# Short remainders of experts taken out of the tile loop into one mixed tile of plain 32-bit matmuls

## The reference

```python
logits = x @ w_gate + modality_bias[modality_id]
e_idx = np.argmax(logits, axis=1)
gate_w = probs[np.arange(N), e_idx]          # softmax of the logits at the chosen expert
for e in range(8):
    mask = e_idx == e
    h = np.maximum(x[mask] @ w1[e], 0.0)     # 512 -> 1024
    out[mask] = gate_w[mask, None] * (h @ w2[e])   # 1024 -> 512
```

## Time and profile before

| | |
|---|---|
| Median of three runs | 540.8 us (538.77 to 544.58) |
| Profiled execution | 541.94 us, its span 540.2 us |
| Mean granted TensorE clock in it | 0.988 of full speed |
| TensorE matmuls busy | 521.1 us, 96% of the span |
| VectorE, ScalarE, GpSimd busy | 40%, 38%, 41% |

### The profile page before, as it was taken

How to read it: one execution, slowest core, us unless ns; L and a number is a source line. 1 busy time by engine, 2 the same in 40 slices (tenths; PEclk the granted TensorE clock), 3 DMA queues, 4 the chain that set the end, 5 groups by cost and what they waited for, 6 DMA issues and landing times. The chain is left out here.

```text
span 540.2 us, 9225 instructions
## 1 busy us (share of the span) xinstructions
PE 521.1 (96%) x3000; PEld 430.0 (80%) x3001; DVE 215.6 (40%) x417; ACT 204.9 (38%) x352; POOL 222.6 (41%) x236
## 2 busy tenths in 40 slices
PE   7899999999999999999999999999989999999994
PEld 6778888888778888878888888878878888888873
DVE  3443332333335422223533566462222472222892
ACT  0143343333343344444334556222222552222880
POOL 2675554554322556444245735041121161112461
PEclk8899999999999999999999999999999999999997
DMA  5954434430020530006400000205873101111110
GB/s 175 400 225 157 147 128 156 152 83 9 0 79 2 184 127 0 0 0 224 165 0 1 0 1 27 91 23 167 261 254 136 39 21 39 39 39 39 39 36 2
DMA packets 23161, 49.54 MB, mean 92 GB/s; under 512 B 8919, under 2 KB 10591, under 8 KB 23136
## 3 DMA queue, kind: packets, MB, share of 16 engines
q1 hardware_dynamic: 16496, 41.83, 21.9%
q0 software_dynamic: 2896, 7.36, 4.4%
q10 hardware_dynamic: 3744, 0.03, 0.4%
HBM read 42.80 MB, written 7.20 MB: 93 GB/s over the span
## 5 line engine op out<-in xcount | busy, mean ns | idle before, releaser
L523 POOL TENSOR_TENSOR wi_lo<-wd_raw,wi_hi 128x512 fp32r<-128x512 f32 x48 | 62.2, 1296 | 145.1 <-ACT wi_hi L670 145.0
L1264 PE MATMUL psum<-xT,wi_lo 128*128 128x512 f32 x192 | 77.3, 402 | 0.0
L1272 PE MATMUL psum<-wo_hi,act_lo 128*128 128x512 f32 x192 | 75.7, 394 | 1.3 <-DVE act_lo L922 1.3
L1266 PE MATMUL psum<-xT,wi_hi 128*128 128x512 f32 x192 | 75.0, 391 | 0.0
L1265 PE MATMUL psum<-xT,wi_hi 128*128 128x512 f32 x192 | 74.9, 390 | 0.0
L1274 PE MATMUL psum<-wo_hi,act_hi 128*128 128x512 f32 x192 | 74.8, 390 | 0.0
L1273 PE MATMUL psum<-wo_lo,act_hi 128*128 128x512 f32 x192 | 74.7, 389 | 0.0
L919 DVE SCALAR_TENSOR_TENSOR act_f<-psum,act_f 128x512 f32<-128x512 f32 x48 | 33.1, 690 | 97.2 <-ACT act_f L688 96.7
L688 ACT ACTIVATE act_f<-psum 128x512 f32<-128x512 f32 x48 | 28.6, 597 | 97.3 <-PE psum L1266 94.1
L528 POOL TENSOR_TENSOR wo_lo<-wd_raw,wo_hi 128x512 fp32r<-128x512 f32 x48 | 61.9, 1289 | 2.7 <-ACT wo_hi L675 2.7
L1353 PE MATMUL psum<-we_hi,he_lo 128*128 128x512 f32 x120 | 48.4, 403 | 2.4 <-DVE he_lo L1013 2.0
(11 more groups left out here) (170 smaller groups left out, 832.3 us busy)
## 6 DMA issues: line engine op xcount, KB each, us to landing
we_raw<-w_exp SPq DMA_DIRECT2D x32, 512.0 KB, 4.9
wd_raw<-w_dense SPq DMA_DIRECT2D x16, 512.0 KB, 5.8
qk_in<-attn_qk SPq DMA_DIRECT2D x10, 512.0 KB, 3.4
kv_in<-attn_kv SPq DMA_DIRECT2D x10, 512.0 KB, 3.4
x_d<-x_sb SPq DMA_DIRECT2D x12, 256.0 KB, 2.3
qk_more<-attn_qk SPq DMA_DIRECT2D x2, 512.0 KB, 7.1
kv_more<-attn_kv SPq DMA_DIRECT2D x2, 512.0 KB, 7.8
decay_mask<-pow_d SPq DMA_DIRECT2D x2, 256.0 KB, 3.6
```

Source lines behind the costliest of these rows:

```text
L523: nc.gpsimd.tensor_tensor(wi_lo[:, r, :], dense_raw(f, 0), wi_hi[:, r, :].bitcast(F32), ALU.subtract).then_inc(s_wil, 1)
L1264: nc.tensor.matmul(h, w_lo, hi, start=(c == 0), stop=False)
L1266: mm = nc.tensor.matmul(h, w_hi, hi, start=False, stop=(c == DC - 1))
L1272: nc.tensor.matmul(bank(ACC + i), lo, wo_hi[:, r, :], start=first, stop=False)
```

## The change

Before the tile table is made, VectorE marks experts whose remainder (the last, partly filled tile) has at most `MR = 32` rows, up to three of them (`MIX = 3`); for the first two experts in the order a mark needs more than one tile in all. Each marked expert gets one tile less. Its remaining rows go to a mixed tile of 3 x 32 rows that always runs once, after the tile loop: `ids_m` holds their tokens and gates, `xg_m` the gathered rows. No operand is split. The raw weights of the three experts are loaded again (or for the first time) into the three buffers of `we_raw`, after the last split of the tile loop has read them. Where fewer than three are marked, the places hold slots of no token and expert 0's weights.

The first layer of expert q runs as 16 products of 256 columns, four at a time in j: each takes 32 rows of tokens as stationary operand and writes PSUM partitions 32j to 32j+31. The second layer runs as 8 x 3 products of 512 columns, where q chooses the 32 partitions. In the table code two steps for tile 0 and 1 (`evacuate_early(0)`, `hid(1, 0)`) are moved ahead of the table's last reduction, and seven steps are added in front of it. The last tile's second half is cut up and its slices stand between the steps of the mixed tile.

With the counts above the order of the experts is 7, 6, 1, 3, and their rows behind the three early tiles are 393, 750, 6 and 3: tiles 4, 6, 1, 1 before. The remainders are 9, 110, 6 and 3 rows, so that experts 7, 1 and 3 are marked and the tiles become 3, 6, 0, 0.

VectorE, in the table code:

```diff
+            nc.vector.tensor_scalar(rem_i[:], cnt_i[:], P - 1, None, ALU.bitwise_and)
             tlink(nc.vector.tensor_copy(n_til, cnt_s[:]))
+            tlink(nc.vector.tensor_tensor(big[:], n_til, kept[:], ALU.is_gt))
+            tlink(nc.vector.scalar_tensor_tensor(out=small[:], in0=rem_i[:], scalar=float(MR), in1=big[:],
+                                                 op0=ALU.is_lt, op1=ALU.mult))
+            tlink(nc.vector.tensor_tensor(s_tri[:], tri[:].rearrange("p a b -> p b a"), by_column(small[:]), ALU.mult))
+            tlink(nc.vector.tensor_reduce(turn_no[:], s_tri[:], AX_X, ALU.add))
+            tlink(nc.vector.scalar_tensor_tensor(out=mixed[:], in0=turn_no[:], scalar=float(MIX), in1=small[:],
+                                                 op0=ALU.is_lt, op1=ALU.mult))
+            tlink(nc.vector.tensor_tensor(n_til, n_til, mixed[:], ALU.subtract))
...
+            nc.vector.tensor_copy(tab_f[:, WHOLE_:WHOLE_ + 1], tab_f[:, LOADS_:LOADS_ + 1]).then_inc(s_tb, 1)
+            tb[0] += 1
+            dve.wait_ge(s_tb, tb[0])
...
+            evacuate_early(0)
+            hid(1, 0)
             tlink(nc.vector.tensor_reduce(tab_f[:, 0:4 * NTAB], val[:].rearrange("p q t e -> p (q t) e"), AX_X, ALU.add))
             nc.vector.tensor_copy(tab[:], tab_f[:]).then_inc(s_tab, 1)
 
 
-            evacuate_early(0)
-            hid(1, 0)
```

Behind that nine more steps fill the small table `m_tab` (for each q the expert and the slot of its remainder) and set `s_mtab`, ahead of `rows_lo(2)`. SyncE, right behind its read of `LOADS_` and ahead of `sp.wait_ge(s_gat, 16 * (PRE + 1))`:

```diff
+            sp.wait_ge(s_mtab, 1)
+            for i in range(2):
+                sp.wait_ge(s_scat[i], 16 * CHUNKS // 2)
+            for q in range(MIX):
+                at = sp.value_load(m_tab[0:1, MIX + q:MIX + q + 1], min_val=0, max_val=SLOTS)
+                sp.dma_start(ids_m[q * MR:(q + 1) * MR, :], slots_d[bass.ds(at, MR), :]).then_inc(s_mids, 16)
```

SyncE, at its end:

```diff
+            sp.wait_ge(s_el, whole * FC2 + FC2)
+            sp.sem_inc(s_pass, 1)
+            for i in range(2):
+                sp.wait_ge(s_el2[i], whole * (FC2 // 2) + FC2 // 2)
+                sp.sem_inc(s_pass, 1)
+            for q in range(MIX):
+                e = sp.value_load(m_tab[0:1, q:q + 1], min_val=0, max_val=E - 1)
+                for f in range(FC2):
+                    if q * FC2 + f >= AHEAD:
+                        before_f = q * FC2 + f - AHEAD
+                        sp.wait_ge(s_mw[before_f % FC2], 16 * (before_f // FC2 + 1))
+                    sp.dma_start(we_raw[:, raw_mix(q), f, :], w_exp[bass.ds(e * FC2 + f, 1)].rearrange("a p n -> p (a n)")
+                                 ).then_inc(s_mw[f], 16)
```

GpSimd, ahead of its tile loop, and after `scatter(last)`:

```diff
+            pool.wait_ge(s_mids, 16 * MIX)
+            pool.indirect_dma_start(out=xg_m[0:MX, :], out_offset=None, in_=x2_d,
+                                    in_offset=bass.IndirectOffsetOnAxis(ap=ids_m[0:MX, 0:1].bitcast(U32), axis=0)
+                                    ).then_inc(s_mgat, 16)
...
+            pool.wait_ge(s_my, 1)
+            pool.indirect_dma_start(out=out, out_offset=bass.IndirectOffsetOnAxis(ap=ids_m[0:MX, 0:1].bitcast(U32), axis=0),
+                                    in_=y_m[0:MX, :], in_offset=None, bounds_check=TOK - 1, oob_is_err=False
+                                    ).then_inc(s_mout, 16)
+            pool.wait_ge(s_mout, 16)
```

ScalarE, after `hid(last, 1)` (`load_ids(ids_s, last)` stands between the two pieces):

```diff
+            act.wait_ge(s_mt, 1)
+            nc.scalar.activation(xT_m[:].rearrange("p c n -> p (c n)"), bank(T_PS)[:, 0:DC * MX], ACT.Copy).then_inc(s_mx, 1)
...
+            for q in range(MIX):
+                act.wait_ge(s_mht, q + 1)
+                nc.scalar.activation(hT_m[:, q, :], bank(MIX_T[q])[:, 0:2 * P], ACT.Relu).then_inc(s_mr, 1)
```

VectorE, after `hid(last, 1)`:

```diff
+            for q in range(MIX):
+                dve.wait_ge(s_mu, q + 1)
+                nc.vector.tensor_copy(h_m[:, q, :], bank(MIX_H[q])[:, 0:2 * P]).then_inc(s_mh, 1)
             evacuate_late(last)
+            dve.wait_ge(s_md, 1)
+            nc.vector.tensor_scalar(y_m[0:MX, :], bank(T_PS)[0:MX, :], ids_m[0:MX, 1:2].bitcast(F32), None, ALU.mult).then_inc(s_my, 1)
```

TensorE, at its end:

```diff
-            down(last, k, 1)
+            pe.wait_ge(s_mgat, 16)
+            for c in range(DC):
+                mm = nc.tensor.transpose(bank(T_PS)[:, c * MX:(c + 1) * MX], xg_m[0:MX, c * P:(c + 1) * P], ident[0:MX, 0:MX])
+            mm.then_inc(s_mt, 1)
+            down(last, k, 1, range(2))
+            def up_mixed(q):
+                for f in range(FC2):
+                    pe.wait_ge(s_mw[f], 16 * (q + 1))
+                for c in range(DC):
+                    for j in range(4):
+                        mm = nc.tensor.matmul(bank(MIX_H[q])[j * MR:(j + 1) * MR, 0:2 * P], xT_m[:, c, q * MR:(q + 1) * MR],
+                                              we_raw[:, raw_mix(q), j // 2 * 4 + c, j % 2 * 2 * P:(j % 2 + 1) * 2 * P],
+                                              start=(c == 0), stop=(c == DC - 1), skip_group_check=True)
+                mm.then_inc(s_mu, 1)
+            def turn_mixed(q):
+                pe.wait_ge(s_mh, q + 1)
+                for u in range(2):
+                    mm = nc.tensor.transpose(bank(MIX_T[q])[:, u * P:(u + 1) * P], h_m[:, q, u * P:(u + 1) * P], ident[:])
+                mm.then_inc(s_mht, 1)
+            pe.wait_ge(s_mx, 1)
+            up_mixed(0)
+            up_mixed(1)
+            turn_mixed(0)
+            up_mixed(2)
+            turn_mixed(1)
+            down(last, k, 1, range(2, 3))
+            turn_mixed(2)
+            down(last, k, 1, range(3, 4))
+            for i in range(FC2):
+                u, j = i // 4, i % 4
+                for q in range(MIX):
+                    if i == 0:
+                        pe.wait_ge(s_mr, q + 1)
+                    mm = nc.tensor.matmul(bank(T_PS)[q * MR:(q + 1) * MR, :], hT_m[:, q, u * P + j * MR:u * P + (j + 1) * MR],
+                                          we_raw[:, raw_mix(q), 2 * j + u, DM:], start=(i == 0), stop=(i == FC2 - 1),
+                                          skip_group_check=True)
+            mm.then_inc(s_md, 1)
```

More of the change, by code:

```diff
@@ L42 @@
 SLOTS = E * TOK
+PAD = P
+MIX = 3
+MR = 32
+MX = MIX * MR
 PWW = 264
@@ L144, in fused_program @@
         val = spare("val", [1, 4, NTAB, E], F32)
+        big = spare("big", [1, E], F32)
+        small = spare("small", [1, E], F32)
+        s_tri = spare("s_tri", [1, E, E], F32)
+        turn_no = spare("turn_no", [1, E], F32)
+        mixed = spare("mixed", [1, E], F32)
+        rem_i = spare("rem_i", [1, E], I32)
+        at_mix = spare("at_mix", [1, MIX, E], F32)
+        row_at = spare("row_at", [1, E], F32)
+        m_val = spare("m_val", [1, 2, MIX, E], F32)
+        place = Placer(dense_off, dense_off + DENSE_W)
+        h_m = place("h_m", [P, MIX, 2 * P], F32)
+        hT_m = place("hT_m", [P, MIX, 2 * P], F32)
+        assert place.off <= dense_off + DENSE_W // 2
+        place = Placer(dense_off + DENSE_W // 2, dense_off + DENSE_W)
+        xg_m = place("xg_m", [P, DM], F32)
+        xT_m = place("xT_m", [P, DC, MX], F32)
+        y_m = place("y_m", [P, DM], F32)
         act_off = share_off + SHARE + XT
@@ L182, in fused_program @@
         t_iota = sb("t_iota", [1, NTAB, E], F32)
+        kept = sb("kept", [1, E], F32)
+        q_iota = sb("q_iota", [1, MIX, E], F32)
+        m_tab_f = sb("m_tab_f", [1, 2 * MIX], F32)
+        m_tab = sb("m_tab", [1, 2 * MIX], I32)
+        ids_m = sb("ids_m", [P, 2], I32)
         e_id = sb("e_id", [1, E], F32)
@@ L198, in fused_program @@
         pre_no = sb("pre_no", [1, 2, E], F32)
-        tab_f = sb("tab_f", [1, 4 * NTAB + 2], F32)
-        tab = sb("tab", [1, 4 * NTAB + 2], I32)
-        SB_, KT_, FI_, ID_, LAST_, LOADS_ = 0, NTAB, 2 * NTAB, 3 * NTAB, 4 * NTAB, 4 * NTAB + 1
+        tab_f = sb("tab_f", [1, 4 * NTAB + 3], F32)
+        tab = sb("tab", [1, 4 * NTAB + 3], I32)
+        SB_, KT_, FI_, ID_, LAST_, LOADS_, WHOLE_ = 0, NTAB, 2 * NTAB, 3 * NTAB, 4 * NTAB, 4 * NTAB + 1, 4 * NTAB + 2
         ids_pre = sb("ids_pre", [P, PRE, 2], I32)
@@ L240, in fused_program @@
         HT = 2
+        MIX_H = (1, MISC, HID)
+        MIX_T = (HT, HT + 1, HID + 1)
         def turn_bank(t, i):
@@ L313, in fused_program @@
         s_out = sem("out_scattered")
+        s_mtab = sem("mixed_table_ready")
+        s_mids = sem("mixed_ids_loaded")
+        s_mgat = sem("mixed_rows_gathered")
+        s_mw = [sem(f"mixed_weights{f}") for f in range(FC2)]
+        s_mt = sem("mixed_rows_transposed")
+        s_mx = sem("mixed_rows_copied")
+        s_mu = sem("mixed_hidden_done")
+        s_mh = sem("mixed_hidden_copied")
+        s_mht = sem("mixed_hidden_transposed")
+        s_mr = sem("mixed_relu_ready")
+        s_md = sem("mixed_rows_summed")
+        s_my = sem("mixed_y_ready")
+        s_mout = sem("mixed_rows_scattered")
         s_pass = sem("wait_passed")
@@ L447, in _ @@
             loads = sp.value_load(tab[0:1, LOADS_:LOADS_ + 1], min_val=RAWS, max_val=E)
+            whole = sp.value_load(tab[0:1, WHOLE_:WHOLE_ + 1], min_val=KNOWN, max_val=E)
+            sp.wait_ge(s_mtab, 1)
[4 more added lines that the diff above has]
```

(19 more changed lines are left out.)

8 lines of the change are left out of this document (5 added, 3 removed).

## The result

The changed kernel takes 521.35 us in the median (520.04 to 521.69, 4 runs), the kernel before 540.9 us beside it: ratio 0.963, 95% interval 0.957 to 0.968, so 19.6 us less. The profiled execution took 520.04 us, its span is 518.3 us.

A forecast was written before the change was run, and what follows sets the result against it. TensorE's stream was taken to set the end. Terms: -38.3 (tiles removed) + 14.5 (mixed tile) + 1.9 (table) + 0.8 (weights) = -21.1 us, so 540.8 becomes 519.7 us in the median's terms; range 515 to 531 for 8 in 10.

The forecast's parts named there:

- What bounds the kernel, and what goes: TensorE's stream sets the end; three tiles fewer in the loop remove 38.3 us.
- The mixed tile: TensorE's added work after the loop: matmuls 12.7 us, with transposes, changes and a wait 14.5 us.
- the rest of it: Mixed tile beside its matmuls: transposes 0.35 and 0.5, array changes 0.5, a last relu wait 0.4 us.
- the one step taken beyond the rows: Mixed tile's matmuls: full overlap, seen for two halves, taken to hold for four quarters (5.4 us) and three (7.3).
- Weight loads hidden: Mixed tile: 144 new weight loads hide beside matmuls; the rival, not hidden, adds 19.7 us, 539.4, chance 0.03.
- The table: Longer table code before the tile loop delays ScalarE's relu and rows: new TensorE wait of 1.9 us (0.5 to 3).
- The two waits that the forecast named: Behind the table, TensorE waits for the relu's end (366.7) and the rows' low part (367.9 to 368.0).
- The weights: 24 raw-weight slices on SP start at 430.5, last lands at 489.5; hidden, 0.8 us for traffic.
- Cover as stated: Mixed tile's weight slices land 10 us before expert q = 2 needs them, unless a slice takes over 2.8 us.
- late slices: Rival: mixed tile's weight slices at 3.3 us each land 11 us after the need, 531 us; chance 0.05.
- I take 0.8 us (0 to 3): Tile loop: allowance for weight slices running beside five tiles' gathers and id loads, 0.8 us.
- also hidden: SP's superfluous load of a third expert was claimed to be hidden.

The follow-up runs named there:

- e13: Changed kernel with all mixed-tile products writing PSUM partitions 0 to 31, overwriting each other, so mixed rows' results are lost: 549.58 us, ratio 1.017 to the kernel before.
- e1: Changed kernel with the mixed tile's products reordered so that products in a row use the same quarter of the array: 538.79 us, ratio 0.997.
- e11: Changed kernel with SP keeping one slice of the mixed tile's weights under way instead of two: 541.8 us, ratio 1.003.
- e2: Changed kernel with the mixed tile's first layer taking its quarters in pairs, second layer unchanged: 520.31 us in one run.
- e9: Changed kernel with the count of weight loads no longer raised to three; the loop still ran once, so the eight slices stayed: 520.6 us, ratio 0.964.
- e12: Changed kernel with SP's loop over further whole experts taken out, right for these inputs only: 516.67 us, ratio 0.956.
- e4: Changed kernel with ScalarE's wait for copied ids and next id load moved behind hid(t, 1), in both loop branches: 518.01 us, ratio 0.958.
- e5: Changed kernel with ScalarE doing relu(1, 1) and rows(2) ahead of its wait for the table: 519.05 us, ratio 0.959.

## Why the prediction was right

Forecast 519.7 us (range 515 to 531), measured 521.35. By its steps:

- *What bounds the kernel, and what goes.* 38.3 us out and 14.5 in were forecast for TensorE's end, -23.8; measured -24.3. The tiles are twelve, as the counts said.
- *The mixed tile.* Up 5.5 (forecast 5.4), down 6.9 (7.3), the rest of it 1.6 (1.8). No row before showed more than two parts of the array side by side. That it goes on to four was the one step taken beyond the rows, and e13 and e1 show that all depends on it. Measured against one quarter alone (e13) the gain is 3.8 times for four and 3.0 for three. By the gains that the Trainium skill gives in "TensorE: Matmul & The Clock Gate", Part 3 (2.38 times for three column tiles, 3.07 for four row tiles), the mixed tile would, as an estimate, be 3.6 us dearer; this trace does not agree.
- *Weight loads hidden.* Held: 0.110 us each, all beside matmuls with the same rows of the array. The Trainium skill states in the same page and part that weight loads overlap running matmuls only where the row groups differ; this trace disagrees, as the one before did.
- *The table.* 1.9 us forecast, 2.5 measured. The two waits that the forecast named, for ScalarE's relu and VectorE's low part of the rows, are 0.88 and 0.55 us, 1.4 in all. A third, of 0.91 us (0.4 before), it did not name: counted from tile 0, VectorE does the two moved steps 0.5 us later than before, since the seven new ones stand in front of them. So the size came out nearer than its parts.
- *The weights.* Start forecast 430.5, measured 431.7; last landing 489.5 against 488.3. That the hours agree so well is luck in part: this execution was at tile 0 3.4 us sooner than the one before, and counted from tile 0 the start came 4.6 us later than forecast. Cover as stated, and e11 shows its price. The reason given for late slices, that they share "DMA rings" with scatters and gathers, is not what the profile shows: the slices are in queue q1, gathers and scatters in q0, ScalarE's id loads in q10 (2880 packets, 0.02 MB), all on the same 16 engines.
- *The mis-sized term* is the last: "I take 0.8 us (0 to 3)" for the traffic beside gathers and id loads. It measured 3.2 us, and not where that step put it. Tiles 6 to 10, beside the 24 slices, lost nothing, although their id loads took 3.3 to 4.9 us to land. The stall that before held 1.38 us grew to 3.02 and drew the lower clock after it (1.6 us more). Part of that size is chance: in the six executions that go through the changed kernel's steps up to there (this one, e1, e2, e9, e11, e13) tiles 3 to 5 took 0.2 to 3.2 us more than in the one of the kernel before, 2.0 in the mean. The step called SP's superfluous load of a third expert "also hidden"; e12 shows that this load is what makes the ids late, and e4 that ScalarE's in-order queue turns a late id load into a stall.
- *Together* -21.1 was forecast, -18.5 found in this pair of profiles apart from the part ahead of the change, -19.6 in the medians.

Open stays whether, and why, the stall is longer than before the change. In those six executions it was 3.02, 3.17, 1.13, 3.11, 0.41 (with 1.35 one tile sooner) and 2.21 us, so it varies; of the kernel before there is only one profile, with 1.38. That the longer table moves the eight slices later against the tiles was not tried by itself.

## What to carry to other kernels

A padded tile costs the same however few rows it holds: 12.3 us here. If several such rests of at most 32 rows can be put on different quarters of TensorE's columns, plain 32-bit products for all of them together (14.0 us for three rests) are cheaper than a tile of split products for each (37.0), provided that neighbours in the stream use different quarters (e1, e13) and their weights are in SBUF in time (e11). Before adding waits behind a table, look at what stands in order behind the waiting instruction on each engine, and at loads that serve nothing: a stall of 2 to 4 us can bring the lower clock and be paid twice.

## What was not expected of the hardware

- TensorE looks ahead over quarters: products of the next quarter start while about four of this one are still queued, so a bad order cost 17.4 us where a single quarter cost 28.
- Instructions for four quarters start 6 to 8 ns apart, then 196 ns pass until the next four (256 columns); for three, 416 ns (512 columns).
- An id load of 1 KB, from its issue to its use, takes 2.5 us without the eight slices of 512 KB close by (e12) and 4.0 to 6.2 us with them, although it has a queue of its own.
- The length of a wait alone does not tell whether it is paid twice. After 3.02 us (changed kernel), 2.21 us (e13) and 3.79 us (e5) without a matmul the next ones came 0.43 us apart for over 3 us. After 3.11 us (e9), 1.38 us (before) and 1.13 us (e2) they came 0.23 us apart at once. What else decides stays open.
